# One score order for every head, a split wait, two first loads and an earlier 320-key transpose, in a fused attention and MLP kernel

## What is computed

```python
scores = scale * np.matmul(q, k.transpose(0, 1, 3, 2))
mask = block_i >= block_j                       # 64 x 64 blocks
attn = softmax(np.where(mask, scores, -1e9))
x = np.matmul(attn, v)
# stage 1: h = relu(x @ w_in); u, v = halves of h; v normalised over its channels,
#          gated = u * (w_spatial @ v + b_spatial); x = gated @ w_out
# stage 2: x + relu(layernorm(x) * g_ln @ w_ch1) @ w_ch2
```

## The kernel before

| columns in a quarter | LOW-HIGH | LOW-LOW | HIGH-HIGH | HIGH-LOW |
|---|---|---|---|---|
| before, heads 0 to 8 | 1088 | 512 | 512 | 768 |
| before, heads 9 to 31 | 832 | 640 | 768 | 640 |
| after, all heads | 800 | 640 | 800 | 640 |

## Time and profile before

### The profile page before, as it was taken

How to read it: one execution, slowest core, us unless ns; L and a number is a source line. 1 busy time by engine, 2 the same in 40 slices (tenths; PEclk the granted TensorE clock), 3 DMA queues, 4 the chain that set the end, 5 groups by cost and what they waited for, 6 DMA issues and landing times.

```text
span 774.3 us, 14021 instructions
## 1 busy us (share of the span) xinstructions
PE 763.8 (99%) x5024; PEld 673.6 (87%) x5024; DVE 476.2 (61%) x963; ACT 365.7 (47%) x970; POOL 389.5 (50%) x508
## 2 busy tenths in 40 slices
PE   7999999999999999999999999999999999999998
PEld 6877899879988899889988899888988998989886
DVE  5776745375553755258777666788566687444435
ACT  4886765546554655332542342543333345333331
POOL 3787665334452335223465555565645457454641
PEclk9999999999999999999999999999999999999999
DMA  7444331312224210040553211003100001300002
GB/s 237 147 167 142 111 114 47 118 47 77 77 61 131 54 68 5 28 150 16 164 148 118 87 55 55 28 0 123 55 28 2 1 0 46 119 1 1 0 1 82
DMA packets 38148, 56.38 MB, mean 73 GB/s; under 512 B 3136, under 2 KB 20544, under 8 KB 38080
## 3 DMA queue, kind: packets, MB, share of 16 engines
q1 hardware_dynamic: 38080, 55.49, 22.3%
HBM read 46.04 MB, written 9.44 MB: 72 GB/s over the span
## 4 chain that ended last, share of the span: by engine, by line
PE 97%; DVE 1%; ACT 1%; issue 1%; POOL 0%; POOLq 0%; ACTq 0%; DVEq 0%
PE psum L1402 25%; PE psum L1403 25%; PE psum L1401 25%; PE psum L1314 7%; PE psum L1363 5%; PE psum L1382 4%; PE psum L1387 3%; PE psum L1367 2%; PE psum L1484 1%; ACT probs L811 1%; PE psum L1453 1%; PE psum L1436 1%; DVE neg_max L1041 1%; PE psum L1434 0%; DVE mix_buf L1103 0%
## 5 line engine op out<-in xcount | busy, mean ns | idle before, releaser
L765 POOL TENSOR_TENSOR wp_r<-block,wp_r 128x256 fp32r<-128x256 f32 x168 | 134.0, 805 | 168.0 <-ACT wp_r L945 165.7
L1218 DVE TENSOR_TENSOR sums<-psum,sums 128x384 f32<-128x384 f32 x216 | 113.7, 554 | 105.6 <-PE psum L1403 104.9
L973 ACT ACTIVATE h_r<-sums 128x384 fp32r<-128x384 f32 x96 | 50.6, 527 | 228.6 <-PE psum L1403 119.0
L697 POOL TENSOR_SCALAR probs<-probs,row_inv 128x64 f32<-128x64 f32 (+4 forms) x160 | 89.3, 579 | 108.2 <-DVE row_inv L1052 108.2
L1403 PE MATMUL psum<-w_r,h_r 128*128 128x512 f32 x288 | 114.2, 397 | 0.0
L1402 PE MATMUL psum<-w_r,h_r 128*128 128x512 f32 x288 | 113.7, 395 | 0.0
L1401 PE MATMUL psum<-operand,wp_r 128*128 128x384 f32 x336 | 113.2, 337 | 0.2 <-DVE sums L1218 0.2
L1402 PE MATMUL psum<-operand,wp_r 128*128 128x384 f32 x336 | 113.0, 336 | 0.0
L1403 PE MATMUL psum<-operand,wp_r 128*128 128x384 f32 x336 | 112.4, 334 | 0.0
L1401 PE MATMUL psum<-w_r,h_r 128*128 128x512 f32 x288 | 111.9, 389 | 0.0
L811 ACT ACTIVATE probs<-psum,neg_max 64x64 f32<-64x64 f32 (+4 forms) x160 | 83.2, 528 | 48.2 <-DVE neg_max L1041 47.5
(11 more groups left out here) (121 smaller groups left out, 1608.1 us busy)
## 6 DMA issues: line engine op xcount, KB each, us to landing
qk_raw<-qk SPq DMA_DIRECT2D x32, 576.0 KB, 4.5
block<-w_ch SPq DMA_DIRECT2D x32, 256.0 KB, 3.8
y_res<-y_scratch SPq DMA_DIRECT2D x18, 256.0 KB, 4.1
out<-y_res SPq DMA_DIRECT2D x18, 256.0 KB, 2.1
v_raw<-vN SPq DMA_DIRECT2D x16, 256.0 KB, 2.8
y_scratch<-mix_buf SPq DMA_DIRECT2D x16, 256.0 KB, 2.0
y_ring<-y_scratch SPq DMA_DIRECT2D x16, 256.0 KB, 2.7
w_raw<-w_in SPq DMA_DIRECT2D x8, 256.0 KB, 4.5
```

The source lines that it names most:

```text
L697: pool.tensor_scalar(probs[:, n % 2, c], probs[:, n % 2, c], row_inv[:, n % 2, AT[t]:AT[t] + 1], 1.0, ALU.mult, ALU.mult).then_inc(normed, 1)
L765: pool.tensor_tensor(wp_lo[:, n % WP], w1[i % BLOCKS][:, WEIGHT[j]], wp_hi[:, n % WP].bitcast(F32), ALU.subtract).then_inc(wp_lo_done, 1)
L1218: dve.tensor_tensor(dst, product_bank(i, j), other, ALU.add).then_inc(c_summed, 1)
```

## The change

```diff
-        def turned_later(n):
+        EARLY_EXPS = 1 + len(WIDE)
+        def own_later(n):
             return 0 <= n < HEADS - 2 and n not in (H, H + 2)
...
+                if n == 0:
+                    for a, landed in enumerate((qk_loaded[0], k_loaded)):
+                        sp.dma_start(qk_raw[:, 0, a, :], qk[0, 0][:, S * a:S * (a + 1)]).then_inc(landed, 16)
+                    return
...
             def score_head(n):
                 pe.wait_ge(q_scaled, n + 1)
-                if n >= 1:
+                if 1 <= n <= H:
+                    pe.wait_ge(exped, NT * (n - 1) + EARLY_EXPS)
+                elif n > H:
                     pe.wait_ge(exped, NT * n)
-                if n > H:
                     pe.wait_ge(t_copied_act, len(ACT_TILES) * (n - 2) + 2)
                 score(n, score_of(n, 0), LOW, 0, slice(0, BLOCK)).then_inc(scored_own, 1)
+                seen(n, 4, LOW, 1).then_inc(scored_wide, 1)
+                seen(n, 4, LOW, 0).then_inc(scored_wide, 1)
+                seen(n, 4, HIGH, 1, start=512, end=KEYS[4]).then_inc(scored_wide, 1)
                 if n <= H:
-                    seen(n, 4, LOW, 1).then_inc(scored_wide, 1)
-                    seen(n, 4, LOW, 0).then_inc(scored_wide, 1)
                     seen(n, 3, HIGH, 0).then_inc(scored_wide, 1)
                     seen(n, 3, HIGH, 1).then_inc(scored_wide, 1)
-                    seen(n, 2, HIGH, 0).then_inc(scored_narrow, 1)
-                    seen(n, 4, HIGH, 1, start=512, end=KEYS[4]).then_inc(scored_wide, 1)
-                    seen(n, 2, LOW, 1, end=256).then_inc(scored_narrow, 1)
-                    seen(n, 1, HIGH, 0).then_inc(scored_narrow, 1)
-                    seen(n, 2, LOW, 1, start=256).then_inc(scored_narrow, 1)
-                    seen(n, 1, LOW, 1).then_inc(scored_narrow, 1)
-                    return
-                seen(n, 2, HIGH, 1, end=256).then_inc(scored_narrow, 1)
+                    if n >= 1:
+                        pe.wait_ge(exped, NT * n)
+                seen(n, 2, HIGH, 1, end=288).then_inc(scored_narrow, 1)
                 seen(n, 2, HIGH, 0).then_inc(scored_narrow, 1)
-                seen(n, 4, LOW, 1).then_inc(scored_wide, 1)
-                seen(n, 4, LOW, 0).then_inc(scored_wide, 1)
-                seen(n, 3, HIGH, 0).then_inc(scored_wide, 1)
-                seen(n, 3, HIGH, 1).then_inc(scored_wide, 1)
+                if n > H:
+                    seen(n, 3, HIGH, 0).then_inc(scored_wide, 1)
+                    seen(n, 3, HIGH, 1).then_inc(scored_wide, 1)
                 pe.wait_ge(scored_narrow, SCORES * n + 2)
                 seen(n, 1, LOW, 0).then_inc(scored_narrow, 1)
-                seen(n, 2, LOW, 1, start=256).then_inc(scored_narrow, 1)
+                seen(n, 2, LOW, 1, start=288).then_inc(scored_narrow, 1)
                 seen(n, 1, LOW, 1).then_inc(scored_narrow, 1)
-                seen(n, 4, HIGH, 1, start=512, end=KEYS[4]).then_inc(scored_wide, 1)
...
-            keep_warm(10)
+            keep_warm(7)
             pe.wait_ge(masks_set, 4)
             pe.wait_ge(consts_set, 5)
+            pe.wait_ge(k_loaded, 16)
             score_head(0)
...
                     if step == 0:
-                        if turned_later(n - 1):
-                            transpose_tile(n - 1, 2)
+                        if own_later(n - 1):
                             transpose_tile(n - 1, OWN)
...
                     elif step == 2:
-                        if not turned_later(n):
-                            transpose_tile(n, 2)
+                        transpose_tile(n, 2)
+                        if not own_later(n):
                             transpose_tile(n, OWN)
```

More of the change, by code:

```diff
@@ L227, in transformer_block @@
         qk_loaded = [sem(f"qk_loaded{s}") for s in range(QS)]
+        k_loaded = sem("k_loaded")
         v_loaded = [sem(f"v_loaded{s}") for s in range(2)]
@@ L893, in _ @@
                 for step in range(STEPS):
-                    if step == 0 and turned_later(n - 1):
+                    if step == 0 and own_later(n - 1):
                         copy_transposed(n - 1, OWN)
@@ L1120, in _ @@
                 for step in range(STEPS):
-                    if step == 0 and turned_later(n - 1):
-                        copy_transposed(n - 1, 2)
                     for b, g in late(n, step, 1):
@@ L1143, in _ @@
                             split_x(b, k)
-                    elif step == 2 and not turned_later(n):
+                    elif step == 2:
                         copy_transposed(n, 2)
```

## The result

The changed kernel takes 784.09 us (median of 4 runs, 783.23 to 784.45) against 775.8 for the kernel before (4 runs, 774.81 to 776.26): a ratio of 1.0107 [1.0095, 1.0120], 8.3 us slower. The sign is the one forecast, but the time lies above 780.7 and above the end of the range.

The account below looks back on a forecast made before the run. TensorE was taken to bound the kernel, busy 763.8 of 774.3 us. Start and early heads -1.6 plus heads 9 to 31 +6.8 gave +5.2 us: 780.7 by the median of 775.46, range 777.5 to 783.0.

Parts of the forecast that it names:

- Then 0.09 to the weight load: 1.28.: Heads 9 to 31: weight load behind the wait for tile 2 starts 0.09 after the 512-column scores end, at 1.28.
- the 0.06 for refilling: Heads 9 to 31: cost of refilling empty quarters, taken as 0.06 between nothing and 0.15; no row shows it.
- +6.8: Heads 9 to 31: scores take 1.87, 20 heads at +0.31 and 3 at +0.20, in us.
- Signals in program order across the quarters: Scores: a signal comes only after those of all scores ahead in the program, so tile 2's can't precede tile 4's.
- The rival with 772.4: Signals come as each quarter finishes; scores of 1.51 in heads 9 to 31, -3.1 in all, 772.4 us; 12%.
- Heads alone: Heads 1 to 8: the same wait is new; scores 2.21 for 1.96, a head 5.39 for 5.23, bound by TensorE.
- The forecast that VectorE hears of the wide scores at 1.16 + 0.09: Heads alone: VectorE is told at 1.16 + 0.09 instead of 1.41, so head 8's exponentials start 0.16 earlier.
- Start: Head 0 scored at 4.92 instead of 6.08, -1.15; head 1 at 10.12 instead of 12.06, -1.94.
- The rival that the start gives little: Low clock lasts longer or q lands no earlier: start and early heads give -0.2, not -1.6; 782.1 us; 12%.
- The moves: Tile 2's transposes go among groups and VectorE's copy ahead of step 2's normalisation, forecast at no cost.
- the rival whose 784.5 lies nearest to the measured time: The move of tile 2 opens waits, VectorE or its copy late, 0.2 us in 19 heads: +9, 784.5; 4%.
- Balance: Heads among groups: by column counts alone, 800 for 832, the change would gain 32 x 1.68 ns = 0.05 a head.

Follow-up runs that it names:

- The runs with five, two and one signals: Changed kernel (784.09 us); in heads 9 to 31 its five wide scores signal once (782.62 us); tile 2's two scores ahead of the wait also signal once (781.44 us).
- one 512 ahead: Changed kernel, but in heads 9 to 31 only tile 4's lower 512-column score, of all long ones, stays ahead of tile 2's scores: 779.27 us.
- tile 2 first: Changed kernel with its 800-column balance, but in heads 9 to 31 tile 2's two scores stand right behind the own score, ahead of tile 4's: 773.87 us.

## Why the prediction was right in sign and wrong in size

**The step that failed** is the first one in the sum for heads 9 to 31: "Then 0.09 to the weight load: 1.28." The 512 columns end at 1.186, as worked out (1.19). But the wait clears 0.227 behind them and not 0.09, which puts the weight load at 1.41. What follows fits in sum: 0.38 + 0.21 = 0.59 from there to the attention, measured 0.59. That is partly luck, since the 0.06 for refilling in it was a choice between 0 and 0.15, and no run shows it by itself. So scores take 2.00 and not 1.87, +0.446 a head and not +0.31. 20 x 0.446 and 3 x 0.34 make +9.9 in place of +6.8. The trace has +9.37 between head 9 and the last attention. Of the rest, 0.18 stands between the scores of heads 9 and 10, and the 2 x 0.22 of the run with tile 2's transposes alone stands behind heads 19 and 27 here too.

**Why 0.227.** The 0.09 was read where only two signals and no longer score stand ahead of the wait. In the new order the first 512-column score holds back everything behind it, and then its own signal and four more come out one after another before TensorE sees the one it waits for. The runs with five, two and one signals clear at 0.227, 0.149 and 0.123 behind the same end: 26 ns a signal. With one 512 ahead (three signals, and behind the long score four held-back passes where the changed kernel has eight) it is 1.217 - 1.076 = 0.141, 0.086 less: two signals are 0.052 of it, which leaves 0.034 for four passes, 8.5 ns each, and 0.227 - 5 x 0.026 - 8 x 0.0085 = 0.029 for the rest. The 26 ns a signal are shown by runs that differ in nothing else; the split of the rest into passes and a fixed part is an estimate from a single run. It holds in lists that it was not made from. Two signals, and the two passes of tile 2's second score behind the end of its first, give 0.029 + 2 x 0.026 + 2 x 0.0085 = 0.098. The traces have 0.801 - 0.702 = 0.099 with tile 2 first, 1.684 - 1.585 = 0.099 in the heads alone, and 0.748 - 0.650 = 0.098 in head 10 of before.

The Trainium skill ("TensorE: Matmul & The Clock Gate", section "The cost: per-tile semaphore tail") states that increments at the end of matmuls serialise, with a tail of 25 + 4.7 for each tile + 26.3 for each increment, in ns. The 26 agrees with these runs. With a held-back pass counted as a tile, it gives 25 + 8 x 4.7 + 5 x 26.3 = 194 ns for the changed kernel, an estimate 0.03 under the 0.227 measured.

**Signals in program order across the quarters**, the premise of the forecast, stands: the wait follows the end of a score in another quarter, whichever stands ahead (1.186 with the upper one, 1.076 with the lower one), and is gone with tile 2 first. The rival with 772.4 needed signals that come as each quarter finishes, and falls. Of the rule that the prediction takes from the Trainium skill (in that page it stands under "The mechanism": matmuls keep program order in start and in end), the trace bears out the part on the ends, as far as the signals tell it; the ends in the trace are modelled. The starts don't keep the order: in head 10 of the changed kernel tile 2's 256-column score starts 0.034 after the start of the scores, and the 288-column one ahead of it in the program at 0.185.

**Heads alone** had the right mechanism too, a little short: tile 2's 288 columns end at 1.585 and not 1.53, the weight load behind them comes at 1.684 and not 1.62, then 0.59, scores 2.275 for 2.21. A head takes 5.46 for 5.39. Over five heads that is most of why head 9 gained 1.1 and not 1.6. The forecast that VectorE hears of the wide scores at 1.16 + 0.09 failed for the same reason as above: it starts at 1.39, since four more signals queue behind the first 512.

**Start**: 4.80 for 4.92, head 1 at 10.11 for 10.12, head 2 at 14.85 for 14.87, head 3 at 20.31 for 20.26. The hit at head 1 is partly luck: the first maximum came 2.39 after the scores' start and not 2.28, which made up for the earlier start, and other kernels with the same start score head 1 as early as 8.92. The rival that the start gives little falls in this trace; by itself, though, the start was worth only 0.4 us in the medians, inside the noise.

**The moves** of tile 2's transposes and its copy open no wait of the size the rival had; by the run with them alone they are worth up to 0.7 in the trace. So the rival whose 784.5 lies nearest to the measured time was wrong in its mechanism, and its number is a coincidence.

**Balance.** "By column counts alone ... 0.05 a head" was wrong as well: measured nothing. The slope of 1.68 ns a column was read between lists that differ by 256 columns, and 32 columns fewer ahead of the last 192-column score don't move its second pass. In every list the attention starts 0.25 behind the start of that pass (1.306 and 1.558, 1.751 and 2.003, 2.022 and 2.275). Why it starts at 1.306 with tile 2 first is open: neither the busiest quarter's columns (832, 800) nor the moment of the wait (0.72, 0.75, 0.80) moves it.

With the measured 2.00 and the measured start of head 9 the sum becomes -1.1 + 9.9 - 0.4 = +8.4, against +8.3 in the medians.

## What to carry to other kernels

When small matmuls share the array, place each one whose result is waited for inside the burst ahead of all long ones in the program, not only ahead in its own quarter, and count a signal for every score that is held back as well. Where such a wait binds, give a signal only to the last of a group that one waiter takes. Balancing 32 columns between quarters was worth nothing here; look first at what order the waits want.

## What the runs showed of the hardware

- Signals at the end of matmuls cost 26 ns each when they are held back behind a longer one (0.227, 0.149, 0.123 us with five, two and one), also where the longer one runs in another quarter, and are free when they aren't waited for: with one fewer ahead of a wait that did not bind, the scores stayed at 1.56.
- A 64 by 64 pass of 32 columns lasts 204 ns, one of 64 columns 229 (ends as modelled); behind two 32-column passes the second 192-column pass starts no earlier than behind two of 64 (1.306 us).
- The first scores of the kernel take 2.10 to 3.64 us from one kernel's profile to the next with nearly the same instructions ahead of them (2.71 before, 3.51 in the changed one); the profile's clock column reads 1.00 in all these stretches, though TensorE's warm-up passes start 0.213 us apart ahead of head 0's scores and 0.112 behind them. The moment at which the pace doubles differs from trace to trace, and with it the start of head 1, by 1.2 us (8.92, 9.12, 10.10 and 10.11 in four kernels with the same start). Shifts of single traces carry this; how far medians do was not measured.
